# Attention, low-rank token mixing and MLP on one core: query tiles of 128, 128, 128, 96 and 96 rows, and batch 0's residuals and turned u packed into three slots

## What is computed

```python
q_rot, k_rot = (rotate(q), rotate(k))
scores = scale * np.matmul(q_rot, k_rot.transpose(0, 1, 3, 2))
scores = scores - np.max(scores, axis=-1, keepdims=True)
attn = np.exp(scores)
attn = attn / (np.sum(attn, axis=-1, keepdims=True) + 1e-09)
attn_out = np.matmul(attn, v)                      # (4, 8, 576, 64)
x = attn_out.transpose(0, 2, 1, 3).reshape(4, 576, 512)
h = x.transpose(0, 2, 1) @ U @ V                   # U (576, 32), V (32, 576)
u = x + h.transpose(0, 2, 1)
out = u + np.maximum(u @ w_ch1, 0.0) @ w_ch2       # (512, 2048), (2048, 512)
```

## Time and profile before

| | us |
|---|---|
| median of 3 runs | 755.5 |
| lowest, highest | 755.38, 759.19 |
| the profiled execution's own time | 755.52 |
| span of its profile, first to last instruction | 753.7 |
| granted TensorE clock, mean | 1.000 |

### The profile page before, as it was taken

The page is one execution under the profiler, slowest core; times in us unless marked ns, Lnnn a source line. Parts: engine busy times, 40 slices in busy tenths (PEclk is TensorE's granted clock), DMA queues, the critical chain, the costliest instruction groups (busy, mean ns, idle before and its releaser), DMA issues.

```text
span 753.7 us, 12305 instructions
## 1 busy us (share of the span) xinstructions
PE 712.1 (94%) x4292; PEld 640.9 (85%) x4292; DVE 407.8 (54%) x676; ACT 438.8 (58%) x948; POOL 465.4 (62%) x338
## 2 busy tenths in 40 slices
PE   3999987899999989999999999899999999999998
PEld 2888875799998879999999988788999889898986
DVE  5799997655556775344444566666555441112111
ACT  2788876676666666565565665667656343434341
POOL 4898865585668664664946867628433346565653
PEclk9999999999999999999999999999999999999999
DMA  7777675537474438348274373462623254434342
GB/s 208 196 210 201 190 208 153 179 95 207 129 228 134 140 126 246 131 144 241 85 220 165 103 209 131 139 191 79 160 70 107 69 196 137 165 128 168 127 167 72
DMA packets 73756, 117.82 MB, mean 156 GB/s; under 512 B 27040, under 2 KB 27168, under 8 KB 71904
## 3 DMA queue, kind: packets, MB, share of 16 engines
q1 hardware_dynamic: 73472, 116.68, 51.2%
q10 hardware_dynamic: 224, 0.36, 0.2%
HBM read 80.15 MB, written 9.44 MB: 119 GB/s over the span
## 4 chain that ended last, share of the span: by engine, by line
PE 75%; DVE 10%; ACT 7%; issue 5%; POOL 1%; DMA 1%; POOLq 0%; SPq 0%; ACTq 0%; DVEq 0%
PE ps L1131 25%; PE ps L1147 23%; PE ps L1045 8%; PE ps L1031 8%; PE ps L1065 6%; DVE negmax L865 3%; ACT prob L711 2%; PE ps L1058 1%; DVE ptl L874 1%; PE ps L1023 1%; ACT pth L722 1%; PE ps L1088 1%; DVE pth L878 1%; DMA raw<-in_qk 1%; PE ps L1113 1%
## 5 line engine op out<-in xcount | busy, mean ns | idle before, releaser
L650 POOL TENSOR_TENSOR w2l<-w2u,w2h 128x512 fp32r<-128x512 f32 x96 | 123.9, 1291 | 227.6 <-ACT w2h L775 227.6
L966 DVE SCALAR_TENSOR_TENSOR htl<-ps,hth 128x384 fp32r<-128x384 f32 x96 | 53.6, 558 | 183.9 <-ACT hth L782 183.6
L865 DVE TENSOR_REDUCE negmax<-ps 128x1 f32<-128x576 f32 (+1 forms) x160 | 120.2, 751 | 54.7 <-PE ps L1031 45.1
L711 ACT ACTIVATE prob<-ps,negmax 128x576 f32<-128x576 f32 (+1 forms) x160 | 117.9, 737 | 35.7 <-DVE negmax L865 34.4
L722 ACT ACTIVATE pth<-ps 128x512 fp32r<-128x512 f32 x156 | 87.5, 565 | 82.7 <-PE ps L1065 80.8
L1131 PE MATMUL ps<-ub,w1h 128*128 128x384 f32 x384 | 132.4, 345 | 2.2 <-DVE utl L957 2.2
L1131 PE MATMUL ps<-ub,w1l 128*128 128x384 f32 x384 | 129.5, 337 | 0.0
L1131 PE MATMUL ps<-utl,w1h 128*128 128x384 f32 x384 | 129.3, 337 | 0.0
L644 POOL TENSOR_TENSOR w1l<-w1u,w1h 128x512 fp32r<-128x512 f32 x96 | 123.7, 1289 | 6.7 <-ACT w1h L771 6.7
L782 ACT ACTIVATE hth<-ps 128x384 fp32r<-128x384 f32 x96 | 47.0, 490 | 136.9 <-PE ps L1131 136.7
L1031 PE MATMUL ps<-stack 128*128 128x288 f32 x620 | 113.3, 305 | 10.0 <-ACT prob L711 9.6
(11 more groups left out here) (81 smaller groups left out, 1127.0 us busy)
## 6 DMA issues: line engine op xcount, KB each, us to landing
w1u<-in_w SPq DMA_DIRECT2D x96, 256.0 KB, 2.6
w2u<-in_w SPq DMA_DIRECT2D x96, 256.0 KB, 2.6
stack<-raw SPq DMA_DIRECT2D x60, 288.0 KB, 4.5
raw<-in_qk SPq DMA_DIRECT2D x14, 1152.0 KB, 5.8
stack<-raw SPq DMA_DIRECT2D x60, 144.0 KB, 4.0
v2u<-in_v SPq DMA_DIRECT2D x16, 320.0 KB, 3.9
ubu<-scratch_u SPq DMA_DIRECT2D x18, 256.0 KB, 3.5
out<-ubu SPq DMA_DIRECT2D x18, 256.0 KB, 2.2
```

The source lines that it names most:

```text
L650: nc.gpsimd.tensor_tensor(w2l[:, at], w2u[:, at], w2h[:, at], ALU.subtract).then_inc(w2_lo, 1)
L711: nc.scalar.activation(tile_of(n, WT[t]).rearrange("p (c n) -> p c n", c=2), scores_of(n, WT[t]), ACT.Exp, bias=negmax[0:WT[t], t:t + 1], ...
L865: nc.vector.tensor_reduce(negmax[0:WT[t], t:t + 1], scores_of(n, WT[t]), AX.XY, ALU.max, negate=True).then_inc(maxed, 1)
```

## The change

The query tiles become 128, 128, 128, 96 and 96 rows (WT), with their first rows in QO; key tiles stay 4 x 128 + 64. Every slice of queries, of rows of x and u and of U and V's tiles goes by QO and WT. Unit 3 has four transposes of 96, TAIL three of 128 and one of 96, LAST five of 96. For batch 3 `pair` does tiles 0 to 2 and `pair_end` tiles 3 and 4.

Batch 0's residuals and turned u, one of each to a slot in slots 52 to 57 before, stand in slots 52 (residual 0, 1, 2), 53 (residual 3, 4, turned_u 0, 1, 2) and 54 (turned_u 3, 4). MLP_FROM goes from 56 to 54: the small ring of banks begins in slot 54, PRIME is slot 53, the weights' first loads stand in slot 50, and the 77 parts of the first region are spread over slots 54 to 92. By the planner that gives `up(0, 0)` in slot 54, `up(0, 1)` in 55, `up(1, 0), up(1, 1), down(0, 0)` in 56 and `down(0, 1), down(0, 2)` in 57; before it was `up(0, 0), up(0, 1)` in 56, none in 57 and `up(1, 0), up(1, 1), down(0, 0)` in 58. From slot 88 on both plans are the same.

```diff
-WT = [min(P, S - P * t) for t in range(NT)]
+KW = S - P * (NT - 1)
+FULL = 3
+WT = [P] * FULL + [(S - P * FULL) // (NT - FULL)] * (NT - FULL)
+QO = [sum(WT[:t]) for t in range(NT)]
+TURNED = QO[NT - 1]
...
-MERGED, LAGGED, MLP_FROM = 46, 51, 56
+MERGED, LAGGED, MLP_FROM = 46, 51, 54
...
-         52: [(0, "residual", 0)],
-         53: [(0, "residual", 1), (0, "turned_u", 0)],
-         54: [(0, "residual", 2), (0, "turned_u", 1)],
-         55: [(0, "residual", 3), (0, "turned_u", 2)],
-         56: [(0, "residual", 4), (0, "turned_u", 3)],
-         57: [(0, "turned_u", 4)],
+         52: [(0, "residual", 0), (0, "residual", 1), (0, "residual", 2)],
+         53: [(0, "residual", 3), (0, "residual", 4), (0, "turned_u", 0), (0, "turned_u", 1), (0, "turned_u", 2)],
+         54: [(0, "turned_u", 3), (0, "turned_u", 4)],
...
-UT_NEEDED = [NT * ((TB * (p + 1) - 1) // S) + ((TB * (p + 1) - 1) % S) // P + 1 for p in range(NB)]
+UT_NEEDED = [NT * ((TB * (p + 1) - 1) // S) + sum(at <= (TB * (p + 1) - 1) % S for at in QO) for p in range(NB)]
...
-REGIONS = ((56, 93, 77), (93, 134, 237), (134, NTILES, 297), (NTILES, SLOTS, 317))
+REGIONS = ((54, 93, 77), (93, 134, 237), (134, NTILES, 297), (NTILES, SLOTS, 317))
...
         if j == TAIL:
-            return bank.rearrange("p (c n) -> p c n", c=1)[0:D], slice(NT - 1, NT), slice(0, BANK)
+            return bank[:, 0:TURNED].rearrange("p (c n) -> p c n", c=1)[0:KW], slice(NT - 1, NT), slice(0, TURNED)
...
-        return bank.rearrange("p (c n) -> p c n", c=NT - 1), slice(0, NT - 1), slice(P * j, P * j + P)
+        return (bank[:, 0:(NT - 1) * WT[j]].rearrange("p (c n) -> p c n", c=NT - 1), slice(0, NT - 1),
+                slice(QO[j], QO[j] + WT[j]))
...
-        rows, tiles = (P, slice(0, NT - 1)) if what == "pair" else (WT[-1], slice(NT - 1, NT))
+        rows, tiles = (P, slice(0, FULL)) if what == "pair" else (WT[-1], slice(FULL, NT))
...
-                        mm = nc.tensor.transpose(bank[:, 0, P * t:P * t + P],
-                                                 prob[:, S * t + P * (NT - 1):S * t + S], ident[:, :])
+                        mm = nc.tensor.transpose(bank[:, 0, QO[t]:QO[t] + WT[t]],
+                                                 prob[0:WT[t], S * t + P * (NT - 1):S * t + S],
+                                                 ident[0:WT[t], 0:WT[t]])
```

More of the change, by code:

```diff
@@ L308, in build @@
         v2u, v2 = sb_over("v2", "v2u", [P, 2, NT, 2, 2, D])
-        prob = sb("prob", [P, NT * S + P - WT[-1]])
+        prob = sb("prob", [P, NT * S + P - KW])
         pth = sb("pth", [P, NT, S], F32R)
@@ L396, in turned @@
         if j == TAIL:
-            return bank.rearrange("p (c n) -> p c n", c=1)[0:D], slice(NT - 1, NT), slice(0, BANK)
+            return bank[:, 0:TURNED].rearrange("p (c n) -> p c n", c=1)[0:KW], slice(NT - 1, NT), slice(0, TURNED)
         if j == LAST:
             return (bank[:, 0:NT * WT[-1]].rearrange("p (c n) -> p c n", c=NT), slice(0, NT),
-                    slice(P * (NT - 1), S))
-        return bank.rearrange("p (c n) -> p c n", c=NT - 1), slice(0, NT - 1), slice(P * j, P * j + P)
+                    slice(TURNED, S))
+        return (bank[:, 0:(NT - 1) * WT[j]].rearrange("p (c n) -> p c n", c=NT - 1), slice(0, NT - 1),
+                slice(QO[j], QO[j] + WT[j]))
     def pt_of(g):
@@ L423, in ut_cols @@
     def ut_cols(b, t):
-        at = S * (b % 2) + P * t
+        at = S * (b % 2) + QO[t]
         return slice(at, at + WT[t])
@@ L488, in store_u @@
                 sp.wait_ge(u_ready, b * NT + t + 1)
-                at = S * b + P * t
+                at = S * b + QO[t]
                 sp.dma_start(scratch_u[at:at + WT[t], :], xn[0:WT[t], t]).then_inc(u_stored, 16)
@@ L762, in mix @@
                     if b >= 2:
-                        act.wait_ge(up_done, FB * ((S * (b - 2) + P * t + WT[t] - 1) // TB + 1))
+                        act.wait_ge(up_done, FB * ((S * (b - 2) + QO[t] + WT[t] - 1) // TB + 1))
                     nc.scalar.activation(uth[:, :, ut_cols(b, t)],
@@ L1023, in scores @@
                             mm = nc.tensor.matmul(ps[0:WT[t], at + c * BANK:at + c * BANK + CH],
-                                                  first[0:D, 0, q, 0, P * t:P * t + WT[t]],
+                                                  first[0:D, 0, q, 0, QO[t]:QO[t] + WT[t]],
                                                   first[0:D, 0, k, 1, CH * c:CH * c + CH],
@@ L1031, in scores @@
                         mm = nc.tensor.matmul(ps[0:WT[t], at + c * BANK:at + c * BANK + CH],
-                                              stack[:, g % HEADS_STACKED, 0, P * t:P * t + WT[t]],
+                                              stack[:, g % HEADS_STACKED, 0, QO[t]:QO[t] + WT[t]],
                                               stack[:, g % HEADS_STACKED, part, CH * c:CH * c + CH],
@@ L1078, in mix @@
                         mm = nc.tensor.transpose(work(tenant, 0, rows, DM)[:, columns(i - tiles.start)],
-                                                 xt_of(b, t)[:, P * i:P * i + rows], ident[:, :])
+                                                 xt_of(b, t)[:, QO[i]:QO[i] + rows], ident[:, :])
                     mm.then_inc(nat_done, 1)
@@ L1085, in mix @@
                     for i in range(NT):
-                        _, tiles, hi, lo = x_parts("pair" if i < NT - 1 else "pair_end", t)
+                        _, tiles, hi, lo = x_parts("pair" if i < FULL else "pair_end", t)
                         for part in (hi, lo):
@@ L1094, in mix @@
                         mm = nc.tensor.transpose(work(tenant, 0, rows, DM)[:, P * c:P * c + P],
-                                                 xt_of(b, c)[:, P * t:P * t + rows], ident[:, :])
+                                                 xt_of(b, c)[:, QO[t]:QO[t] + rows], ident[:, :])
                     mm.then_inc(nat_done, 1)
@@ L1106, in mix @@
                     pe.wait_ge(h_ready, all_of(HIDDENS, b))
-                    mm = nc.tensor.matmul(work(tenant, 0, rows, DM), vs[:, P * t:P * t + rows], hs[:, :],
+                    mm = nc.tensor.matmul(work(tenant, 0, rows, DM), vs[:, QO[t]:QO[t] + rows], hs[:, :],
                                           start=True, stop=True)
@@ L1200 @@
     vp = np.ascontiguousarray(vp.reshape(B * PAIRS, NT, P, 2, D).transpose(0, 2, 1, 3, 4))
-    u4 = np.zeros((SP_, 4, R), moe_U.dtype)
-    u4[:S] = moe_U[:, None, :]
-    u4 = np.ascontiguousarray(u4.reshape(NT, P, P).transpose(1, 0, 2))
+    u4 = np.zeros((P, NT, 4, R), moe_U.dtype)
+    for t in range(NT):
+        u4[:WT[t], t] = moe_U[QO[t]:QO[t] + WT[t], None, :]
+    u4 = u4.reshape(P, NT, P)
     v4 = np.ascontiguousarray(np.concatenate([moe_V] * 4, axis=0))
```

## The result

| | before | after |
|---|---|---|
| median, us | 755.56 (4 runs) | 750.09 (4 runs, 749.89 to 750.26) |
| ratio, 95% interval | | 0.9917 (0.9892 to 0.9941) |
| span of the profile | 753.7 | 748.5 |
| granted TensorE clock, mean | 1.000 | 0.993 |

What follows compares the result with a forecast made beforehand. The prediction took DVE as fullest in attention-only slots, a round through PE, DVE and ACT in slots 52 to 57, and PE from 141.50 on. Sum: 755.5 - 0.7 (packing) + 0 (tiles) = 754.8 us, range 751.0 to 757.3.

Steps and rivals of the forecast that it cites:

- Part 1, the packing: Slots 52 to 57: earlier residuals, turned u and MLP fill PE waits, but one long stop replaces them; 0.7 us gained.
- maxima forecast at 123.6 and 129.3: Starts on DVE of the row maxima of slots 53 (123.6, was 122.41) and 54 (129.3).
- slot 58 at 145.1: Time the new kernel reaches slot 58, against 145.8 for the old kernel at equal work.
- Part 2: Tiles of 96: columns per head unchanged on every engine; PE's transposes -1.2 to +1.2 us over 20 heads, taken as 0.
- Its ends: PE prices per transpose bracketing 96 rows: 0.35 / 4 = 0.088 us for 128 and 0.50 / 5 = 0.100 for 64.
- The text's own sign for it: In the new profile, four transposes of 96 should take between 0.35 and 0.40 us.
- The attention-only slots: Slots at 54.15 to 71.50, DVE fullest: period to stay 17.35 us for two heads; a move would show the forecast wrong.
- The faster one: Rival: the stop in slot 54 doesn't come, stops of about 4.8 us in slots 54 to 56 go; 750.0, chance 0.12.
- The slower one: Rival: TensorE's clock falls in slot 54; half of some 12 us of matmuls at 1.9 times adds 5.4: 760.2, chance 0.06.
- the 1.12 us at 18.36: Time of four transposes early on, against 0.60 at 117.99; cited for the clock rival as at the lower level.
- The rival of the 96 pieces: PE's 96-row transposes cost either end of their bracket: 753.6 cheap, 756.0 dear, both within 0.5%; chance 0.14.
- The rival in which the packing changes nothing: Slots 55 to 58 stall for banks 6 and 7 as before: 755.5, chance 0.06.

Runs made afterwards that it cites:

- experiments 4 and 5: Kernel before plus one unused 128-row transpose a head, in the middle of LAST's 64-row transposes (763.16, ratio 1.0082) or behind the last one (758.96, ratio 1.0034).
- experiments 3 to 5: First of them: kernel before with LAST's five transposes taken over 96 rows, 754.66 us, ratio 0.9964; the others are experiments 4 and 5.

## Why the prediction was wrong

**Part 1, the packing, held.** Slot by slot: maxima forecast at 123.6 and 129.3, found at 123.56 and 129.10; unit 3 at 129.5 behind a stop of 3.5 us, found at 129.33 behind 3.34; slot 58 at 145.1, found at 145.62; 0.7 us gained, found 0.2 by slot 58 in the first profile and 0.8 in the second, both at a lowered clock (117.50 to 145.16 is 27.66, where the kernel before needs 24.15 + 4.29 = 28.44), and not distinguishable from nothing in the run with the packing alone. Reading the order of each queue off the code and filling in durations from the rows was enough for the steps. That slot 58 also came out so near is in part luck, since the working had the full clock and the clock fell.

**The step that failed is Part 2's "I take the middle, 0, since the piece lies between its neighbours".** Its ends, 0.088 and 0.100 us a piece, were groups divided by their counts, and the 0.100 was taken as the price of a small piece. It was the price of a small piece (0.06, experiments 4 and 5) and of leaving 64 rows again, and the 0.08 us of entering was in the row of the scores ahead, where I did not look. A piece of 96 costs 0.36 / 5 = 0.072, below both ends. The ends were no bounds because they mixed a price by size with a price by change of shape. That is 0.17 of the 0.28 a head, and experiments 3 to 5 show it. The other 0.11 is plain size, read from rows alone: unit 3 and TAIL, eight pieces one behind the other, took 0.80 / 8 = 0.100 each, more than the 0.088 of the text, and 0.69 / 8 = 0.086 after, five of them 32 columns narrower. Together 0.28 over 20 heads, 5.6 us, against -1.2 to +1.2 in the text. The clue was in the trace of before, in the weight loads shown above: 1.9 us of idle "issue" ahead of the 60 loads with 64 rows and none ahead of 200 with 128, in a stretch where PE is otherwise full.

The text's own sign for it, four transposes of 96 between 0.35 and 0.40, was missed too: they take 0.33 (302.66 to 302.99). The attention-only slots, held to stay at 17.35 for two heads, took 17.20, a small gain that the text had not counted. And the range's high end was put at 757.3 where its own sum gives 757.5; nothing hangs on that.

**The rivals.** The faster one named 750.0, and the time was 750.09, by another cause: its stop in slot 54 came. That agreement is luck. The slower one's mechanism came too: the clock fell after the stop. Its 1.9 times was right for matmuls: `up(0, 0)` took 2.06 us (130.71 to 132.77) where two such parts had taken 2.19 at 1.00. What was off is the extent, 0.7 to 1.6 us measured on the path for 5.4 in the text: PE worked at the lower level from 129.33 to 134.9 only, and DVE and ACT set part of the pace there. (Whether the lower level made the 1.12 us at 18.36, as the text takes it, isn't shown: the view from 11 to 19 us gives a granted clock of 1.00.) The Trainium skill's rule cited there (idle gaps throttle the engine; TensorE: Matmul & The Clock Gate) was borne out by the granted clock of 0.50 behind the stop, and by 1.00 once the stop was filled. The rival of the 96 pieces had 1.2 us at its cheap end, where the rows show 5.6. The rival in which the packing changes nothing is not ruled out: the ratio with the packing alone is 1.0006, though the steps that the forecast named came.

## What to carry to other kernels

Ask of every tile size whether it changes the number of rows that TensorE's weights take, and price the change of shape apart from the columns: read a group's cost from the start of the work ahead of it to the start of the work behind it. An even split of the remainder (96 and 96 in place of 128 and 64), or padding a 64-row piece to 96 rows, can be faster with the same or more columns. And where a queue's order leaves a long stop on TensorE, look at the granted clock behind it; a few idle matmuls in the stop can pay (12 of them here).

## What the hardware showed that was not expected

- Going from 128 rows to transposes with 64 and back costs PE about 0.31 us (0.85 against 0.54 in experiments 4 and 5), and ordinary matmuls with 64 rows show it as well (0.21 and 0.20 between starts for 0.11); going to 96 rows and back costs nothing that a row shows. The Trainium skill, TensorE: Matmul & The Clock Gate ("LDWEIGHTS"), says a load's time goes by its columns and not by its rows. The loads agree, 138 and 140 ns; the gap ahead of them does not go by columns. Its section "Step-by-step: what each phase is for" says that loads are pulled ahead of running matmuls where the row groups don't conflict or where the load goes to a background buffer. No run here shows which condition fails with 64 rows.
- The clock also fell at the earlier stop, ahead of slot 52 (1.99 us in both profiles of the changed kernel), in some executions and not in others: 0.73 between 118 and 124 us in the first profile, 1.00 in the second. The kernel before has the like: 40 of 68 executions had a mean granted clock under 1.00 and took 757.0 us or more, and where in them the clock fell isn't shown, since its profile is of one with 1.00.
